# Expert routing of a Fourier transform and two mixture-of-experts layers: three of the limits and two of the token lists move into the first expert stage

## What is computed

```python
X = np.fft.fft(np.fft.fft(x, axis=1), axis=2).real   # 9984 tokens of 256
# first mixture of experts, 8 experts, capacity 9984 / 8 = 1248
logits = x @ w_gate
for idx in np.argsort(-logits.flatten()):            # pairs of token and expert, best first
    tok, e = idx // E, idx % E
    if assigned[tok] >= 0 or counts[e] >= cap: continue
    assigned[tok] = e; counts[e] += 1
out[mask_e] = relu(x[mask_e] @ w1[e]) @ w2[e]
# second mixture of experts: each token goes to its argmax expert, no capacity
out[mask_e] = gate_w * eom * (relu(x[mask_e] @ w1[e]) @ w2[e])
```

## Time and profile before

| | |
|---|---|
| median of three runs | 1447.0 us (1446.63, 1447.0, 1447.99) |
| the profiled execution, its own time | 1448.4 us |
| its span in the trace | 1446.6 us |
| mean granted clock of TensorE | 0.899 of full |
| PE busy | 1291.4 us, 89% of the span |
| PE weight loads (PEld) busy | 1194.7 us |
| DVE busy | 702.1 us, 49% |
| POOL busy | 551.7 us, 38% |
| ACT busy | 336.5 us, 23% |
| chain of work that ended last | PE 75%, DVE 8%, issue 2%, POOL, ACT and DMA 1% each |

### The profile page before, as it was taken

How to read it: one execution, slowest core, us unless ns; L and a number is a source line. 1 busy time by engine, 2 the same in 40 slices (tenths; PEclk the granted TensorE clock), 3 DMA queues, 4 the chain that set the end, 5 groups by cost and what they waited for, 6 DMA issues and landing times.

```text
span 1446.6 us, 31150 instructions
## 1 busy us (share of the span) xinstructions
PE 1291.4 (89%) x10763; PEld 1194.7 (83%) x10764; DVE 702.1 (49%) x1991; ACT 336.5 (23%) x840; POOL 551.7 (38%) x556
## 2 busy tenths in 40 slices
PE   5899657666389999999999999699999999999996
PEld 4567557665179998999989998699999999999996
DVE  2723677776744445444554344634343443343332
ACT  0102100000523333333333233112222222222221
POOL 2800230000035656566564754331344142444411
PEclk9999755555579999999999999799999999999998
DMA  9604620101012221232222222131122222222110
GB/s 346 213 1 152 221 89 31 60 31 60 1 34 92 79 79 62 78 98 77 74 66 79 82 71 77 39 103 44 37 100 73 73 69 73 70 81 95 45 40 23
DMA packets 70726, 116.21 MB, mean 80 GB/s; under 512 B 7784, under 2 KB 50545, under 8 KB 70640
## 3 DMA queue, kind: packets, MB, share of 16 engines
q1 hardware_dynamic: 46864, 72.40, 14.9%
q0 software_dynamic: 11808, 31.03, 6.5%
q10 hardware_dynamic: 11968, 11.63, 2.9%
HBM read 81.87 MB, written 34.45 MB: 80 GB/s over the span
## 4 chain that ended last, share of the span: by engine, by line
PE 75%; DVE 8%; issue 2%; POOL 1%; ACT 1%; DMA 1%; POOLq 0%; DVEq 0%; ACTq 0%
PE bank L869 22%; PE bank L871 22%; PE bank L870 21%; DVE arena L1283 3%; PE bank L799 3%; PE bank L808 3%; PE bank L863 1%; PE bank L950 1%; ACT hot_q L1036 1%; POOL weights_low L575 1%; PE bank L849 1%; DVE hot_r L1448 1%; DVE arena L1290 0%; DVE hot_q L1449 0%; DVE arena L1302 0%
## 5 line engine op out<-in xcount | busy, mean ns | idle before, releaser
L869 PE MATMUL bank<-weights_high,hT_high 128*128 (+1 forms) x1328 | 387.1, 292 | 2.5 <-DVE hT_low L1676 2.5
L870 PE MATMUL bank<-weights_low,hT_high 128*128 (+1 forms) x1328 | 379.3, 286 | 0.0
L871 PE MATMUL bank<-weights_high,hT_low 128*128 (+1 forms) x1328 | 379.2, 286 | 0.0
L869 PE MATMUL bank<-xT_high,weights_high 128*128 128x256 f32 (+1 forms) x1072 | 334.6, 312 | 2.3 <-DVE xT_low L1664 1.3
L871 PE MATMUL bank<-xT_high,weights_low 128*128 128x256 f32 (+1 forms) x1072 | 332.0, 310 | 0.0
L870 PE MATMUL bank<-xT_low,weights_high 128*128 128x256 f32 (+1 forms) x1072 | 331.1, 309 | 0.0
L869 PEld LDWEIGHTS bank<-weights_high,hT_high 128*128 128x128 f32 x1328 | 251.2, 189 | 2.8 <-issue 2.8
L871 PEld LDWEIGHTS bank<-weights_high,hT_low 128*128 128x128 f32 x1328 | 251.5, 189 | 0.0
L870 PEld LDWEIGHTS bank<-weights_low,hT_high 128*128 128x128 f32 x1328 | 250.8, 189 | 0.0
L869 PEld LDWEIGHTS bank<-xT_high,weights_high 128*128 128x128 f32 x1072 | 204.4, 191 | 16.8 <-DVE hT_low L1495 3.2
L871 PEld LDWEIGHTS bank<-xT_high,weights_low 128*128 128x128 f32 x1072 | 203.3, 190 | 11.3
(11 more groups left out here) (232 smaller groups left out, 1446.7 us busy)
## 6 DMA issues: line engine op xcount, KB each, us to landing
arena<-middle ACTq DMA_DIRECT2D x44, 258.0 KB
spectrum<-arena SPq DMA_DIRECT2D x39, 256.0 KB, 2.2
arena<-in_w2a_t SPq DMA_DIRECT2D x8, 1024.0 KB, 5.1
raw<-in_w1a SPq DMA_DIRECT2D x8, 1024.0 KB
raw<-in_w2a SPq DMA_DIRECT2D x8, 1024.0 KB
raw<-in_w1b SPq DMA_DIRECT2D x8, 1024.0 KB
raw<-in_w2b SPq DMA_DIRECT2D x8, 1024.0 KB
arena<-in_x SPq DMA_DIRECT2D x4, 768.0 KB, 4.9
```

The costliest lines, as they stand in the source:

```text
L869: pe.matmul(out_, a[0], b[0], start=start, stop=False)
L870: pe.matmul(out_, a[0], b[1], start=False, stop=False)
L871: return pe.matmul(out_, a[1], b[0], start=False, stop=stop)
```

## The change

The serial part keeps four of the seven phases (`SERIAL`), and the first list only for four slots of expert, 40 tiles. The rest is written into the engines' programs of the first expert stage, at numbered tiles (80 tiles, 0 to 79):

- Limits of phases 4, 5 and 6 at tiles 0 to 9, 10 to 19 and 30 to 39, with a single compare of 128 x 2496 instead of four chunks. In part 0 DVE names and compares; PE counts after the result matmuls of parts 1, 3, 5 and 7, and moves inside those of parts 2, 4, 6 and 8; the count of the taken tokens comes after part 8's. The eighth expert is named and counted at tile 40, the flag is formed at tile 41.
- The list of slots 4 and 5 begins at tile 20, that of slots 6 and 7 at tile 42. Each has positions one tile later, then one-hots in ten pieces of eight columns at tiles 22 to 31 and 44 to 53, with `hot_q` of 20 columns; PE multiplies a piece inside the next tile's result, DVE adds it to a sum and forms rows and tokens at tiles 32 and 54.
- All three lists use a ring of four batches (`RING`) instead of two.
- Experts are worked on in the order in which they close. DVE writes the order, and SP and POOL read each slot's expert from it into a register. SP fetches the first expert's weights once its number is there.
- `w2_t` has two buffers. PE's gate matmuls are in parts: two parts after each round's move and eight after the taken tokens' count, two experts in a phase.
- The read of the flag is behind the whole stage. With 1 the slow search, the full list and all of the stage run again; this code is a second copy of the stage in every engine's program, with semaphores of its own (`Redo`).

The core of the diff:

```diff
+RING = 4
+SERIAL = 4
+LISTS = ((0, 4), (4, 6), (6, 8))
+BATCHES = -(-(N // P) // HOTS)
+LIMIT_AT = {0: 4, 10: 5, 30: 6}
+FINAL_AT = 40
+LIST_AT = {20: 1, 42: 2}
...
+COUNT_STEPS, MOVE_STEPS = (1, 3, 5, 7), (2, 4, 6, 8)
...
             def turned_weights(e):
...
+                if e >= 2:
+                    sp.wait_ge(s_gates_ps, e - 1)
+                sp.dma_start(w2_t[e % 2], w2a_t[e].rearrange("(c p) f -> p c f", p=P)).then_inc(s_w2t[e % 2], 16)
...
+            def expert_of(slot):
+
+                sp.wait_ge(s_order, slot + 1)
+                sp.sem_inc(s_hold, 1)
+                return sp.value_load(order_i[0:1, slot:slot + 1], min_val=0, max_val=E - 1)
...
             turned_weights(0)
-            weights(0, 0, w1a, w2a)
             turned_weights(1)
-            weights(1, 1, w1a, w2a)
+            weights(m1, 0, expert_of(0), w1a, w2a)
             for e in range(2, E):
                 turned_weights(e)
-
-            def expert(e, more):
-                if more:
-                    weights(e + 2, e + 2, w1a, w2a)
-                else:
-                    weights(e + 2, e + 2 - E, w1b, w2b)
-
-            for g in range(0, E // 2 - 1):
-                expert(g * 2, True)
-                expert(g * 2 + 1, True)
-            expert(E - 2, False)
-            expert(E - 1, False)
+            for slot in range(1, E):
+                weights(m1, slot, expert_of(slot), w1a, w2a)
...
+            def gate_part(n):
+
+                e, f = n // FCH, n % FCH
+                if f == 0:
+                    pe.wait_ge(s_w2t[e % 2], e // 2 * 16 + 16)
+                    if e >= 2:
+                        pe.wait_ge(s_gates, e - 1)
+                at_ = f * LG
+                for c in range(DCH):
+                    mm = pe.matmul(bank[3 + e % 2][:, at_:at_ + LG], w2_t[e % 2][:, c, f * P:(f + 1) * P], wgate2[:, c, :],
+                                   start=(c == 0), stop=(c == DCH - 1))
+                if f == FCH - 1:
+                    mm.then_inc(s_gates_ps, 1)
+
+            def above_count(ph, r):
...
+            for ph in range(SERIAL):
                 for r in range(ROUNDS):
-                    above_count(ph * ROUNDS + r)
+                    above_count(ph, r)
+                    move(ph, r)
+                    for f in range(FCH // ROUNDS):
+                        gate_part(ph * 2 * FCH + r * (FCH // ROUNDS) + f)
                 new_count(ph, ind8)
-                gate_rows(ph)
...
+            def route_count(n):
+
+                ph, part = limit_at(n)
+                if part in COUNT_STEPS:
+                    r = COUNT_STEPS.index(part)
+                    route_read(s_pass, ph * ROUNDS + r + 1)
+                    above_count(ph, r)
+                if part == MOVE_STEPS[-1]:
+                    route_read(s_closed, ph - SERIAL + 1)
+                    new_count(ph, ind8)
+                if n == FINAL_AT:
+                    route_read(s_closed, E - 1 - SERIAL + 1)
+                    new_count(E - 1, hot8)
+                if n in LIST_AT:
+                    route_read(s_prefixed, LIST_AT[n])
+                    prefix(bank[7][:, 160:160 + E], LIST_AT[n] + 1, s_pre)
+
...
+                        if fast and f == 2:
+                            route_piece(t)
+                        if fast and f == 4:
+                            route_move(t)
...
+                                    for g, (a, _) in enumerate(LISTS):
+                                        if g and a == e + 1:
+                                            pool.wait_ge(m.row, g + 1)
...
+                            if fast:
+                                g, piece = piece_at(e * TPE + FIRSTS[gi] + j)
+                                if g is not None:
+                                    for c in range(piece * PIECE, min((piece + 1) * PIECE, NT1)):
+                                        lanes(g, c, 2 * TPE)
...
+            for ph in range(SERIAL):
+                src = open_log if ph else log8
+                name(link, src)
+                for r in range(ROUNDS):
+                    compare(ph, r)
+                    if ph and r == 0:
+                        slots(link, ph - 1)
+                    mark(ph, r)
+                    step(link, ph, r)
+                accept(link, ph)
+                counted_new(link, ph)
+                subtract(link, ph)
+                if ph + 1 < SERIAL:
+                    shut(link, src)
+            slots(link, SERIAL - 1)
...
+            def routing(n):
+
+                link = on_limit.link
+                g, piece = piece_at(n)
+                if g is not None:
+                    for j in range(piece * PIECE, min((piece + 1) * PIECE, NT1)):
+                        one_hots(g, j, 2 * TPE)
+                g, piece = piece_at(n - 1)
+                if g is not None:
+                    dve.wait_ge(s_hot_used, g * BATCHES + min((piece + 1) * (PIECE // HOTS), BATCHES))
+                    sums = acc[:].rearrange("p (o q) -> p o q", o=2)
+                    if piece == 0:
+                        link(dve.tensor_copy(sums, list_at()))
+                    else:
+                        link(dve.tensor_tensor(sums, sums, list_at(), ALU.add))
+                    dve.sem_inc(s_added, 1)
+                    if piece == PIECES_OF_LIST - 1:
+                        rows(link, sums, *LISTS[g])
+                        dve.sem_inc(m1.row, 1)
+                        tokens(link, *LISTS[g])
+                if n - 1 in LIST_AT:
+                    positions(link)
+                if n in LIST_AT:
+                    g = LIST_AT[n]
+                    dve.wait_ge(s_given, LISTS[g][0] + 3 if g < len(LISTS) - 1 else E)
+                    running(link)
+                    slot_base(link, g)
+                    dve.wait_ge(s_pre, g + 1)
+                    link(dve.tensor_tensor(quota[:], quota[:], bank[7][:, 160:160 + E], ALU.add))
+                    dve.sem_inc(s_prefixed, 1)
+                ph, part = limit_at(n)
+                if part == 0:
+                    name(link, open_log)
+                    compare(ph, 0)
+                if part in MOVE_STEPS:
+                    r = MOVE_STEPS.index(part)
+                    step(link, ph, r)
+                    if r + 1 < ROUNDS:
+                        compare(ph, r + 1)
+                    else:
+                        accept(link, ph)
+                        counted_new(link, ph)
+                if part in COUNT_STEPS:
+                    mark(ph, COUNT_STEPS.index(part))
+                if part == TPE - 1:
+                    subtract(link, ph)
+                    slots(link, ph)
+                    if ph == E - 2:
+                        expert_of(link, E - 1)
+                    else:
+                        shut(link, open_log)
+                if n == FINAL_AT:
+                    shut(link, open_log)
+                    name(link, open_log)
+                    link(dve.tensor_scalar(new_b[:, 0:NT1], taken[:, 0:NT1], 0.0, None, ALU.is_gt))
+                    dve.tensor_tensor(hot8[:], hot8[:], each_e(new_b), ALU.mult).then_inc(s_new, 1)
+                    counted_new(link, E - 1)
+                if n == FINAL_AT + 1:
+                    dve.tensor_scalar(surs[:, E * E:E * E + E], alone[:], 1.0, None, ALU.not_equal)
+                    link(dve.tensor_tensor(surs[:, (E - 1) * E:E * E], cnt[:], left[:], ALU.subtract))
+                    link(dve.tensor_reduce(move[:], surs, AX.X, ALU.max))
+                    dve.tensor_scalar(flag[:], move[:], 0.0, None, ALU.is_gt).then_inc(s_flag, 1)
+                    dve.wait_ge(s_given, E)
+                    link(dve.tensor_tensor(A, A, hot8[:].rearrange("p j e -> p e j"), ALU.add))
```

1114 lines of the change are left out of this document (660 added, 454 removed).

## The result

The change makes the kernel slower: 1482.8 us, median of four runs (1482.41 to 1487.89), against 1447.5 us before. The ratio is 1.0253, with a 95% interval of 1.0229 to 1.0276. Forecast were 1440.9 us and a range from 1412 to 1466.

What follows compares the result with a forecast made beforehand. It took 164 to 412 us as a chain of waits and 412 to 903 us as bound by PE. 1446.6 - 84.2 + 34 + 40 + 4.1 gave 1440.5, on the medians' scale 1440.9 us, 80% range 1412 to 1466.

Steps and rivals of the forecast that it cites:

- three phases, phase 0 and 1, the way to the list, the list: Serial stretch before the expert stage: three phases leave, waits and list shorten, phase 1 pays; in sum -84.2 us.
- PE's new work in the stage: First expert stage: counts, new-counts, moves and list matmuls now run on a full PE, +34 us, between 20 and 40.
- DVE's lateness: First expert stage: PE waits where DVE's limit and list work comes late, +40 us, between 15 and 62.
- The wait for the third matrix: Phase 1 of the search: PE waits for the third turned w2, issued behind the first expert's weights, +10.5 us.
- What DVE's new work does to PE: Step pricing DVE's late arrivals in the first expert stage, place by place: together +40 us.
- The upper end: First expert stage: each POOL split meets an awaited DVE instruction and such runs double, 62 us of lateness.
- The lower end: First expert stage: no POOL split meets an awaited DVE instruction, 15 us of lateness.
- The clock was a rival: First expert stage: PE's clock falls at the twelve counts, adding 28 us, 1468 us in all; chance 0.05.
- Tile 40: First expert stage: closing, naming and mask make the new-count late, 7 us with PE resuming at half clock.
- tiles 30 to 33: First expert stage: one-hots, naming, compare, rows and tokens crowd DVE, about 12 us of lateness over four tiles.
- the list matmuls: First expert stage, twenty list tiles: the loop through DVE and ACT outlasts PE's tile in about 12, 15 us.
- the lock's mechanism: First expert stage: DVE and POOL take turns, instruction by instruction, wherever POOL splits, 1464.5 us; chance 0.25.

Runs made afterwards that it cites:

- b_counts_scatter: The kernel before with twelve added bursts of 78 count matmuls in the stage, and POOL's first-group scatters moved from index 4 to 6: 1474.8 us.
- light_splits: The changed kernel with POOL's weight splits of slots 2 to 7 cut to 8 columns of each block, most weights stale: 1435.5 us.
- gated5: w2_first with POOL's splits held until a hidden part of PE has begun, five at index 3 and three at index 5: 1462.6 us.
- b_waits: The kernel before with PE waiting for dummy DVE chains behind tiles 6 and 8 of six experts, a count behind each tile 8 wait: 1613 us.
- b_folds: The kernel before with the later steps of the transform's folds that the change brought: 1440.2 us.
- folds_back: The changed kernel with the transform's folds put back at their former steps: 1483.5 us.
- b_folds_ring: The kernel before with the later folds and a ring of four batches of one-hots in place of two, all seven limits serial: 1433.9 us.
- b_counts: The kernel before with twelve bursts of 78 count matmuls added in the stage, waiting for nothing late: 1492.7 us.
- w2_first: The changed kernel with the third and fourth turned matrices issued ahead of the first expert's weights in SP's queue: 1469.9 us.

## Why the prediction was wrong

By the steps of the text, from the two profiles:

| step | forecast | measured |
|---|---|---|
| three phases, phase 0 and 1, the way to the list, the list | -84.2 | -85.8 |
| transform | nothing | -7.8 |
| PE's new work in the stage | +34 | +38 to 40 |
| DVE's lateness | +40 | +60 idle (4 of it stalls inside counts), and 25 to 27 at half clock |
| flag and branches, from the last result to the end | +4.1 | +3.3 |

The serial part was right in sum and in each term: phase 0 gave back 8.1 us (7.7), phase 1 paid 15.9 (5.5 + 10.5), the way from the taken tokens to the first one-hot gained 8.5 (8.2) and the list 8.1 (7.3). The wait for the third matrix was there as described. On the price of a count the row stood (2.2 us, also at full clock, in b_counts_scatter). The Trainium skill (TensorE: Matmul & The Clock Gate, "Wait — 56ns, not 53.3ns?") gave an estimate of 1.95 us; since its 25 ns are a least spacing, and 2.2 us are 28 ns a matmul, the two do not contradict each other.

The step that failed is "What DVE's new work does to PE": +40 us stood there, and the stage paid 85 (60 idle, 25 at half clock). The text's own sign of being wrong, idle time over 60 us, just did not show (59.7); the half clock was in none of its signs. It failed in three ways.

- **The lock was averaged away.** The text had the doubled compares and L1300 and took the middle between "no split meets an awaited instruction" and "each does". The upper end had been reckoned with a factor of two, from a compare of 0.7 us beside a split of 1.3. A one-hot of 0.24 us that is held by that split costs five times its own, and the one-hots are 312 of the new instructions. The idle time alone was 60 us, near the upper end of 62, and 39 to 44 us of the whole hang on the splits (light_splits). The lower end was too low as well: with the splits cut from tile 10 on (light_splits) PE still loses 25.0 us idle and some 10 at half clock, and not 15. That is near the forecast's +40, for which the text had needed half of the lock. The Trainium skill (SBUF — State Buffer, "Who interferes with whom") has this lock for DVE instructions with two SBUF inputs or in a two-port mode: gated5 agrees, with 1.21 us for a small subtraction of two SBUF operands and an unchanged 0.42 for the instruction with a PSUM operand.
- **The clock was a rival and not a term.** The text priced it as twelve falls at the counts, as an alternative to lateness, with a chance of 0.05. It fell eleven times, mostly behind waits. A place that stands for some 4 us cost another 3 in b_waits, so lateness and clock rise together: 60 + 27, where each rival held only one of the two (62, or 40 + 28).
- **Gathers do lock, a little.** The text said that gathers and scatters don't, from one row. The one-hot at 577.66 lasts 0.67 us, to the very end of the gather at 577.33; so did L1546 in the earlier trace rows. Of 49 one-hots beside gathers 42 stayed under 0.4 us, most at 0.25, and all 49 together took 14.7 us (12.3 at 0.25 each). Beside scatters 10 of 64 took 0.4 to 0.5 us. It is small here, and nowhere near the 20 us to which the prediction worked out the Trainium skill's rule for the 16-bit one-hots.

Tile 40 was right (7 us, measured 7.4), tiles 30 to 33 had 12 of lateness for 14.8 of idle time, with half clock on top, and the list matmuls 15 for 26.5: there the locked one-hots are. And one edit of the diff, the folds, was not priced at all, though it was worth 8 us in the other direction in b_folds. So the other terms together are some 50 us off and not 42. That the total was not further off is luck, and so is that folds_back itself took only 1483.5: its counts had no stalls.

Of the rivals, the lock's mechanism was the true one (1464.5), and the clock's on top of it makes the difference to 1482.8.

## What to carry to other kernels

Work that moves off a serial chain into a full stage has to be priced by the place where it is awaited, with the durations that its instructions have beside the other engine that is busy there, and not with those it had alone. Where POOL works on SBUF, count a small DVE instruction with two SBUF operands, and here a 16-bit one-hot too, at the length of POOL's instruction as the upper price; about half of the one-hots beside splits paid it. Each wait of 4 to 20 us that held PE in the full stage brought 1.5 to 2.9 us more at half clock behind it (b_waits): price that too. And look at the small edits of a large change one by one: here a line of five numbers and a deeper ring took 13 to 15 us off by themselves (b_folds_ring), and the changed kernel is 49 us above the kernel that has only these.

## What was not expected of the hardware

- The lock moves with the splits: in gated5 three of them in a hidden part slow the 0.2 us instructions there to 0.6 to 1.2 us, and PE waits 2.7 us behind.
- A gather of 1.0 us holds a one-hot only in its last part (0.67 us, from 577.66 to 578.33).
- PE stands still within a run of 78 small matmuls, mostly for 0.45 to 0.55 us at a time and up to five times a count, in three tiles of b_counts, and does not once POOL's four scatters are elsewhere (1492.7 against 1474.8 us). In w2_first, folds_back and light_splits the same scatters did nothing, so a second condition is open.
